# Four H banks in turn for the first four chunks of block 1, and up-projection (1,4) issued ahead of down-projection (1,0)

## The chip, the cores and the metric

One core of one Trainium2 chip runs the whole program. The metric is the device time of one execution in microseconds (us), of which less is better. The kernel is written for the separate engines of the core: PE (TensorE, matrix products into PSUM), DVE (VectorE), ACT (ScalarE), POOL (GpSimd, which reads and writes SBUF only here) and SP (SyncE, which issues the DMAs). Each engine works through its own list of instructions in order, and they meet at semaphores.

## The reference

Attention over channels is followed by two feed-forward networks (FFNs) over 6016 tokens of 256 channels, with a hidden width of 2048 in both.

```python
s = kn.transpose(0, 2, 1) @ qn / tau          # 256 x 256, softmax of its rows -> a
x = v @ a                                     # 6016 x 256
h = x @ w_in1                                 # first FFN
P = a0 + a1*h + a2*h**2 + a3*h**3
Q = 1 + abs(b0)*abs(h) + abs(b1)*h**2
x = (P / (Q + 1e-6)) @ w_out1
h = x @ w_in2                                 # second FFN
out = (h * clip(h + 3, 0, 6) / 6) @ w_out2
```

## The kernel before

**Tiling.** The tokens are cut into 12 blocks: 11 of 512 tokens and a last one of 384. The hidden width of 2048 is cut into 16 chunks of 128. A pair such as (1,4) is block 1, chunk 4. The softmax result is folded into the first FFN's up weights, so that the first FFN starts from v itself. Each product is made of three matmuls (high by high, high by low, low by high half of the operands, lines 476 to 478), for each of two halves of 128 channels, so one up- or down-projection of a chunk is a group of six matmuls.

**The four groups.** `up1(t, j)` makes a chunk of the first FFN's hidden layer in a bank of the PSUM tensor H. ACT makes the terms of Q and the start of P from it (`q_terms`, lines 804 and 806; `p_start`, line 812). DVE goes on with P in place in the same bank (`horner_2`, line 999; `horner_1`, line 1006), then makes the high half of the quotient (`quotient_hi`, line 1014), a product (`product`, line 1034) and the remainder (`rest`, line 1042). `rest` is the last to read the H bank, and its semaphore `rest_done` sets the bank free. ACT takes the reciprocal root and squares it between (`root`, line 819, and `root_squared`, line 825), after POOL has added up Q (`q_body`, line 423). POOL makes the low half (`quotient_lo`, line 429), for which `down1` (into the PSUM tensor YP) waits. When all 16 chunks of a block are down, `yT_split` (ACT line 846, then DVE line 1060) copies YP to SBUF as two halves, and only then may `down1` of the next block write YP. For the second FFN `up2(b, j)` writes H, `c1` (ACT, line 831), `gate2` (DVE, line 1048) and `c2` (ACT, line 838) read it, POOL splits the result (line 437), and `down2` adds it up in OP.

**Order.** All engines walk through slots (t, j), 16 slots for each block. In slot (t, j) PE issues `up2` of chunk j - 4 of block t - 1, `down2` two chunks behind that, `up1(t, j)`, and `down1` of the chunk three before j. The order is fixed in the program. In slots (1,0) to (1,3) there is no second FFN yet; `up2(0,0)` comes in slot (1,4), and `down2(0,0)` in slot (1,6). The one exception before is slot (1,2), where `down1(0,15)` goes ahead of `up1(1,2)`. On ACT a slot (1, j) with j of 4 and more runs `c1`, `root` and `root_squared` of chunk j - 1, `q_terms`, `p_start`, `c2`. On DVE it runs `gate2`, `quotient_hi`, `product` and `rest` of chunk j - 1, then `horner_2` and `horner_1` of chunk j. Slot (1,3) has `yT_split(0)` at its start on both.

**The H banks.** H has four banks, 0 to 3. In block 0 `up1` takes all four in turn. From block 1 on `up1` takes banks 0 and 1, and `up2` banks 2 and 3. Who waits for which bank stands in `wait_h1` and `wait_h2`; these two, `h1` and `step` of PE are what the change touches. Before, `up1(1,2)` waits for `rest(1,0)`, `up1(1,3)` for `rest(1,1)`, and `up2(0,0)` and `up2(0,1)` for `rest(0,14)` and `rest(0,15)`.

Of the kernel before, what the change touches and what calls it, by code (L numbers as in the profile page):

```python
# [28 lines left out]
def attention_ffn_ffn(nc, q, k, v, tau, w_in1, w_out1, a, b, w_in2, w_out2, out):  # L29
# [3 lines left out]
    J = F // P  # L33
# [18 lines left out]
    LAG_DOWN1 = 3  # L52
# [44 lines left out]
    with ctx:  # L97
# [75 lines left out]
        def first_folded(i, c):  # L173
# [27 lines left out]
        g1_hi_done, product_done, rest_done, g1_lo_done, d1_done = map(  # L201
            sem, ("g1_hi_done", "product_done", "rest_done", "g1_lo_done", "d1_done"))
# [11 lines left out]
        def width(blk):  # L214
            return P * (tiles_of[blk] if isinstance(blk, int) else BT)
# [5 lines left out]
        def exists(blk):  # L221
            return not isinstance(blk, int) or 0 <= blk < NB

        def chunk(t, at):

            return t + at // J, at % J

        def count(blk, j):

            return blk * J + (j + 1)  # L230

        def back(blk, j, n):

            blk, j = blk + (j - n) // J, (j - n) % J
            return None if isinstance(blk, int) and blk < 0 else (blk, j)

        def wait_chunk(engine, semaphore, at):
            if at is not None:
                engine.wait_ge(semaphore, count(*at))
# [20 lines left out]


        def h1(t, j):
            turn = 4 if isinstance(t, int) and t == 0 else 2
            return H[:, j % turn, 0:width(t)]

        def wait_h1(engine, t, j):
            if isinstance(t, int) and t == 0:
                if j >= 4:
                    wait_chunk(engine, rest_done, (0, j - 4))
            elif isinstance(t, int) and t == 1 and j < 2:  # L270
                wait_chunk(engine, rest_done, (0, J - 4 + j))
            else:
                wait_chunk(engine, rest_done, back(t, j, 2))

# [2 lines left out]

        def wait_h2(engine, blk, j):
            if isinstance(blk, int) and blk == 0 and j < 2:
                wait_chunk(engine, rest_done, (0, J - 2 + j))  # L280
            else:
                wait_chunk(engine, g2_done, back(blk, j, 2))

# [12 lines left out]
        def slot(t, j):  # L296
            return t * J + j if isinstance(t, int) else None

        def stage(t, at):

            blk, j = chunk(t, at)
            return (blk, j) if exists(blk) else None
# [170 lines left out]
        def _(pe):  # L473
            def split_product(psum, w_hi, w_lo, x_hi, x_lo, first, last):

                nc.tensor.matmul(psum, w_hi, x_hi, start=first, stop=False)  # L476
                nc.tensor.matmul(psum, w_hi, x_lo, start=False, stop=False)  # L477
                return nc.tensor.matmul(psum, w_lo, x_hi, start=False, stop=last)  # L478
# [71 lines left out]
            def fold_first(i, c):  # L550
                for d in range(CT):
                    done = nc.tensor.matmul(first_folded(i, c), probT[:, d, c * P:(c + 1) * P],
                                            w_raw_a[:, d, i * P:(i + 1) * P], start=(d == 0), stop=(d == CT - 1))
                done.then_inc(first_made, 1)
# [26 lines left out]
            def up1(t, j, par):  # L581
                w = width(t)
                wait_h1(pe, t, j)
                if j == 0:
                    pe.wait_ge(vT_lo_done, CT * (t + 1))
                cols = slice(j * P, (j + 1) * P)
                for c in range(CT):
                    if isinstance(t, int) and t == 0 and j < 2:
                        pe.wait_ge(first_lo, CT * j + c + 1)
                    elif isinstance(t, int) and t == 0 and j in PIECE_AT:  # L590
                        pe.wait_ge(fold_lo, PIECE_AT.index(j))
                    done = split_product(h1(t, j), wf_hi[:, c, cols], wf_lo[:, c, cols],
                                         vT_hi[par][:, c, 0:w], vT_lo[par][:, c, 0:w], c == 0, c == CT - 1)
                done.then_inc(u1_done, 1)

            def down1(blk, j):
                w = width(blk)
                wait_chunk(pe, g1_lo_done, (blk, j))
                if j % 4 == 0 and isinstance(blk, int) and blk == 0:
                    pe.wait_ge(wd1_lo_done, j // 4 + 1)  # L600
                for d in range(CT):
                    if j == 0 and exists(blk - 1):
                        pe.wait_ge(yT_lo_done, CT * (blk - 1) + d + 1)
                    done = split_product(YP[:, d, 0:w], wd1_hi[:, j, d * P:(d + 1) * P],
                                         wd1_lo[:, j, d * P:(d + 1) * P], g1_hi[:, j % 4, 0:w],
                                         g1_lo[:, j % 4, 0:w], j == 0, j == J - 1)
                done.then_inc(d1_done, 1)

            def up2(blk, j):
                w = width(blk)  # L610
                wait_h2(pe, blk, j)
                if isinstance(blk, int) and blk == 0 and j in (0, J // 2):
                    pe.wait_ge(wu2_lo_done, 4 if j == 0 else 8)
                cols = slice(j * P, (j + 1) * P)
                for c in range(CT):
                    if j == 0:
                        pe.wait_ge(yT_lo_done, CT * blk + c + 1)
                    done = split_product(h2(blk, j), wu2_hi[:, c, cols], wu2_lo[:, c, cols],
                                         yT_hi[:, c, 0:w], yT_lo[:, c, 0:w], c == 0, c == CT - 1)
                done.then_inc(u2_done, 1)  # L620
# [70 lines left out]
            def step(t, par):  # L691
                for j in range(J):
                    if x := stage(t - 1, j - SHIFT2):
                        up2(*x)
                    if x := stage(t - 1, j - SHIFT2 - LAG_DOWN2):
                        if isinstance(x[0], int) and x[0] == NB - 1:
                            down2_by_tokens(*x)
                        else:
                            down2(*x)
                    last_of_0 = slot(t, j) == J + LAG_DOWN1 - 1  # L700
                    if last_of_0:

                        down1(0, J - 1)
                    if exists(t):
                        up1(t, j, par)
                        if slot(t, j) == 0:

                            pe.wait_ge(probT_scaled, 1)
                            fold_first(1, 1)
                        if isinstance(t, int) and t == 0 and j in PIECE_AT[:-1]:  # L710
                            fold(PIECE_AT.index(j) + 1)
                    if not last_of_0 and (x := stage(t, j - LAG_DOWN1)):
                        down1(*x)

            every_step(pe, step)
# [422 lines left out]
```

## Time and profile before

| | |
|---|---|
| median of three runs | 1111.23 us (1110.48 to 1111.71) |
| profiled execution, device time | 1110.4 us |
| its span, first to last instruction | 1108.6 us |
| PE busy | 1093.8 us, 99% of the span |
| DVE, ACT, POOL busy | 895.8, 866.3 and 776.1 us |
| chain of work that ended last | PE 92%, DVE 4%, all else under 2% each |

The profile is one execution. Its page has the busy time of each engine, the span in 40 slices with the granted clock of PE, and the chain that ended last; the trace behind it has every instruction with its start, its length, and what ended the idle time before it. Times in the trace are counted from the start of the span. Matmuls overlap: each is shown with some 0.39 us, but the next one starts about 0.23 us after it. So the start of the next group is where a group ends for PE, and the end of its last matmul is where others may read the result. DVE, ACT and POOL instructions overlap a little too, when nothing is waited for between them.

### The profile page before, as it was taken

The page shows a single profiled execution, that of the slowest core. Times are in us where ns is not written, and L with a number is a line of the kernel's source. Part 1 is how long each engine was busy: PE and PEld are TensorE (multiplying, and loading weights), DVE is VectorE, ACT ScalarE, POOL GpSimd, SP SyncE. Part 2 cuts the span into 40 slices and gives each one's busy share as a digit, 9 for nine tenths or more (in the row PEclk, how much of TensorE's full clock was granted, in tenths as well). Part 3 has the DMA queues.
Part 4 walks back from the last instruction along what each step waited for, and adds up shares of the span by engine and source line. Part 5 has one row for each costly group of instructions (what it writes and reads, how often), then busy time and mean ns, then how long its engine had stood idle before and what let it go on. Part 6 is the DMA issues. An engine that isn't in the chain of part 4 may idle for free.

```text
span 1108.6 us, 15700 instructions
## 1 busy us (share of the span) xinstructions
PE 1093.8 (99%) x4966; PEld 914.2 (82%) x4966; DVE 895.8 (81%) x1288; ACT 866.3 (78%) x1461; POOL 776.1 (70%) x624
## 2 busy tenths in 40 slices
PE   9999799999999999999999999999999999999998
PEld 8877588888888888888888888888888888888888
DVE  6799988888888788798788788788888888877742
ACT  6799878877877877787787788788787787777744
POOL 0489878777677777777777667777777767776653
PEclk9999999999999999999999999999999999999999
DMA  9941000011011011011011011002001001001010
GB/s 348 321 119 20 0 16 5 1 20 20 1 20 20 1 20 20 1 19 19 0 19 19 1 20 20 1 2 35 3 1 20 15 1 20 0 2 20 1 20 15
DMA packets 105472, 33.92 MB, mean 31 GB/s; under 512 B 92982, under 2 KB 98742, under 8 KB 105398
## 3 DMA queue, kind: packets, MB, share of 16 engines
q1 hardware_dynamic: 104960, 32.65, 11.8%
q8 instruction: 33, 0.54, 0.2%
q14 instruction: 41, 0.34, 0.1%
q10 hardware_dynamic: 438, 0.39, 0.1%
HBM read 26.87 MB, written 6.16 MB: 30 GB/s over the span
## 4 chain that ended last, share of the span: by engine, by line
PE 92%; DVE 4%; POOL 1%; issue 1%; ACT 0%; DMA 0%; SPq 0%; DVEq 0%; ACTq 0%
PE H L476 15%; PE H L477 15%; PE H L478 15%; PE OP L477 7%; PE OP L478 7%; PE OP L476 7%; PE YP L476 7%; PE YP L477 7%; PE YP L478 7%; PE OP L507 3%; DVE H L1006 1%; DVE T L999 1%; DVE g_hi L1014 1%; DVE SQ L1042 1%; PE OP L676 1%
## 5 line engine op out<-in xcount | busy, mean ns | idle before, releaser
L423 POOL TENSOR_TENSOR SQ<-SQ,AB 128x512 f32<-128x512 f32 (+1 forms) x175 | 224.2, 1281 | 251.2 <-ACT SQ L806 251.2
L437 POOL TENSOR_TENSOR g_lo<-R,g_hi 128x512 fp32r<-128x512 f32 (+1 forms) x191 | 243.6, 1275 | 23.7 <-ACT g_hi L838 22.6
L429 POOL TENSOR_TENSOR g_lo<-SQ,Y 128x512 fp32r<-128x512 f32 (+1 forms) x192 | 245.0, 1276 | 8.6 <-DVE SQ L1042 7.9
L804 ACT ACTIVATE AB<-H,absb 128x512 f32<-128x512 f32 (+1 forms) x175 | 118.9, 680 | 145.3 <-PE H L478 145.2
L999 DVE TENSOR_TENSOR T<-T,H 128x512 f32<-128x512 f32 (+1 forms) x192 | 129.0, 672 | 80.0 <-ACT T L812 79.5
L1014 DVE SCALAR_TENSOR_TENSOR g_hi<-H,coef,Y 128x512 fp32r<-128x512 f32 (+1 forms) x192 | 141.5, 737 | 57.6 <-ACT Y L825 57.2
L476 PE MATMUL YP<-g_hi,wd_hi 128*128 128x512 f32 (+1 forms) x384 | 149.3, 389 | 4.7 <-POOL g_lo L429 4.3
L476 PE MATMUL H<-vT_hi,wf_hi 128*128 128x512 f32 (+1 forms) x384 | 149.2, 388 | 4.8 <-DVE wf_lo L969 2.5
L831 ACT ACTIVATE R<-H 128x512 f32<-128x512 f32 (+1 forms) x192 | 113.5, 591 | 50.4 <-PE H L478 50.4
L1048 DVE SCALAR_TENSOR_TENSOR R<-R,H 128x512 f32<-128x512 f32 (+1 forms) x192 | 128.1, 667 | 29.8 <-ACT R L831 28.3
L1006 DVE SCALAR_TENSOR_TENSOR H<-T,coef,H 128x512 f32<-128x512 f32 (+1 forms) x192 | 143.0, 745 | 6.8
L478 PE MATMUL H<-vT_hi,wf_lo 128*128 128x512 f32 (+1 forms) x384 | 148.0, 385 | 0.0
L478 PE MATMUL H<-yT_hi,wu_lo 128*128 128x512 f32 (+1 forms) x384 | 147.9, 385 | 0.0
L812 ACT ACTIVATE T<-H,coef 128x512 f32<-128x512 f32 (+1 forms) x192 | 147.9, 770 | 0.0
L477 PE MATMUL H<-yT_lo,wu_hi 128*128 128x512 f32 (+1 forms) x384 | 147.9, 385 | 0.0
L477 PE MATMUL H<-vT_lo,wf_hi 128*128 128x512 f32 (+1 forms) x384 | 147.8, 385 | 0.0
L478 PE MATMUL YP<-g_hi,wd_lo 128*128 128x512 f32 (+1 forms) x384 | 147.8, 385 | 0.0
L477 PE MATMUL YP<-g_lo,wd_hi 128*128 128x512 f32 (+1 forms) x384 | 147.8, 385 | 0.0
L476 PE MATMUL H<-yT_hi,wu_hi 128*128 128x512 f32 (+1 forms) x384 | 147.8, 385 | 0.0
L1042 DVE SCALAR_TENSOR_TENSOR SQ<-H,coef,SQ 128x512 f32<-128x512 f32 (+1 forms) x192 | 142.0, 740 | 6.7 <-POOL SQ L417 0.5
L1034 DVE SCALAR_TENSOR_TENSOR SQ<-SQ,g_hi 128x512 f32<-128x512 f32 (+1 forms) x176 | 139.1, 791 | 6.1
L477 PE MATMUL OP<-g_lo,wd_hi 128*128 128x512 f32 x352 | 137.0, 389 | 0.0
(123 smaller groups left out, 2070.8 us busy)
## 6 DMA issues: line engine op xcount, KB each, us to landing
qk<-in_q SPq DMA_DIRECT2D x22, 256.0 KB, 5.6
qk<-in_k SPq DMA_DIRECT2D x22, 256.0 KB, 6.3
out<-o_tok SPq DMA_DIRECT2D x88, 64.0 KB, 1.9
v_blocks<-in_v SPq DMA_DIRECT2D x80, 64.0 KB, 2.3
wd_raw<-in_moe_w_out SPq DMA_DIRECT2D x8, 512.0 KB, 8.2
wu_raw<-in_moe_w_in SPq DMA_DIRECT2D x4, 512.0 KB, 8.0
w_raw_a<-in_moe_w_in SPq DMA_DIRECT2D x2, 1024.0 KB, 10.7
v_blocks<-in_v SPq DMA_DIRECT2D x1, 512.0 KB, 6.8
```

The source lines that it names most:

```text
L423: nc.gpsimd.tensor_tensor(SQ[:, j % 4, 0:w], SQ[:, j % 4, 0:w], AB[:, j % 2, 0:w], ALU.add)\
L429: nc.gpsimd.tensor_tensor(g1_lo[:, j % 4, 0:w], SQ[:, j % 4, 0:w], Y[:, j % 2, 0:w], ALU.mult)\
L437: nc.gpsimd.tensor_tensor(g2_lo[:, j % 4, 0:w], R[:, j % 2, 0:w], g2_hi[:, j % 4, 0:w].bitcast(fp32), ALU.subtract).then_inc(g2_lo_done, 1)
L476: nc.tensor.matmul(psum, w_hi, x_hi, start=first, stop=False)
L477: nc.tensor.matmul(psum, w_hi, x_lo, start=False, stop=False)
L478: return nc.tensor.matmul(psum, w_lo, x_hi, start=False, stop=last)
L812: nc.scalar.activation(T[:, j % 2, 0:w], h1(t, j), ACT.Identity, bias=A2, scale=A3)\
L999: nc.vector.tensor_tensor(T[:, j % 2, 0:w], T[:, j % 2, 0:w], h1(t, j), ALU.mult)\
L1006: nc.vector.scalar_tensor_tensor(h, T[:, j % 2, 0:w], A1, h, ALU.add, ALU.mult).then_inc(t3_done, 1)
L1014: nc.vector.scalar_tensor_tensor(g1_hi[:, j % 4, 0:w], h1(blk, j), A0, Y[:, j % 2, 0:w], ALU.add, ALU.mult).then_inc(g1_hi_done, 1)
L1034: nc.vector.scalar_tensor_tensor(SQ[:, j % 4, 0:w], SQ[:, j % 4, 0:w], Q_CONST, g1_hi[:, j % 4, 0:w].bitcast(fp32), ALU.add, ALU.mult).the ...
L1042: nc.vector.scalar_tensor_tensor(SQ[:, j % 4, 0:w], h1(blk, j), A0, SQ[:, j % 4, 0:w], ALU.add, ALU.subtract).then_inc(rest_done, 1)
```

## The change

The first FFN keeps four H banks in turn for chunks 0 to 3 of block 1 too. So `up1(1,2)` and `up1(1,3)` write banks 2 and 3, and wait for `rest(0,14)` and `rest(0,15)`. `up1(1,4)` and `up1(1,5)` write banks 0 and 1 again, and wait for `rest(1,0)` and `rest(1,1)`. `up2(0,0)` and `up2(0,1)`, whose banks are 2 and 3, now wait for `rest(1,2)` and `rest(1,3)`. On PE `up1(1,4)` moves from slot (1,4) to slot (1,3), between `up1(1,3)` and `down1(1,0)`, and the exception of slot (1,2) is gone: `up1(1,2)` goes ahead of `down1(0,15)`. The other engines' lists are what they were, but for the bank that they address; no instruction is added or taken away.

```diff
         def h1(t, j):
-            turn = 4 if isinstance(t, int) and t == 0 else 2
+            turn = 4 if isinstance(t, int) and (t == 0 or (t == 1 and j < 4)) else 2
             return H[:, j % turn, 0:width(t)]
 
         def wait_h1(engine, t, j):
             if isinstance(t, int) and t == 0:
                 if j >= 4:
                     wait_chunk(engine, rest_done, (0, j - 4))
-            elif isinstance(t, int) and t == 1 and j < 2:
+            elif isinstance(t, int) and t == 1 and j < 4:
                 wait_chunk(engine, rest_done, (0, J - 4 + j))
+            elif isinstance(t, int) and t == 1 and j < 6:
+                wait_chunk(engine, rest_done, (1, j - 4))
             else:
                 wait_chunk(engine, rest_done, back(t, j, 2))
...
         def wait_h2(engine, blk, j):
             if isinstance(blk, int) and blk == 0 and j < 2:
-                wait_chunk(engine, rest_done, (0, J - 2 + j))
+                wait_chunk(engine, rest_done, (1, 2 + j))
             else:
                 wait_chunk(engine, g2_done, back(blk, j, 2))
...
-                    last_of_0 = slot(t, j) == J + LAG_DOWN1 - 1
-                    if last_of_0:
-
-                        down1(0, J - 1)
-                    if exists(t):
+                    if exists(t) and slot(t, j) != J + 4:
                         up1(t, j, par)
...
-                    if not last_of_0 and (x := stage(t, j - LAG_DOWN1)):
+                    if slot(t, j) == J + 3:
+
+                        up1(t, 4, par)
+                    if x := stage(t, j - LAG_DOWN1):
                         down1(*x)
```

## Rows read from the trace of the kernel before

**Rows 1.** The page, granted TensorE clock in 40 slices of the span, in tenths.

```profile
PEclk9999999999999999999999999999999999999999
```

**Rows 2.** Waits of PE over the whole span: total us, times, longest us.

```profile
PE YP L476 <- POOL g_lo L429: 4.3, 5, 1.7
...
PE H L476 <- DVE SQ L1042: 2.3, 1, 2.3
```

**Rows 3.** Stretch from 134.2 us on: length, then busy us of PE, PEld, DVE, ACT, POOL.

```profile
134.20:1108.00 973.80, 970.92 (x4410) 814.16 (x4410) 781.75 (x1117) 752.22 (x1286) 696.41 (x559) 1.00 0.07 12
```

**Rows 4.** PE's timeline, slots (1,1) to (1,5): start us, length us, line, operation, [idle before].

```profile
117.52 0.40 PE L478 MATMUL YP<-g_hi,wd_lo 128*128 128x512 f32 x1
119.65 0.50 PE L476 MATMUL YP<-g_hi,wd_hi 128*128 128x512 f32 x1 [1.73 <-POOL g_lo L429]
...
121.17 0.39 PE L476 MATMUL H<-vT_hi,wf_hi 128*128 128x512 f32 x1
...
124.97 0.50 PE L476 MATMUL H<-vT_hi,wf_hi 128*128 128x512 f32 x1 [2.29 <-DVE SQ L1042]
...
127.04 0.47 PE L476 MATMUL YP<-g_hi,wd_hi 128*128 128x512 f32 x1 [0.41 <-DVE yT_lo L1060]
...
128.50 0.40 PE L476 MATMUL H<-yT_hi,wu_hi 128*128 128x512 f32 x1
...
129.65 0.39 PE L478 MATMUL H<-yT_hi,wu_lo 128*128 128x512 f32 x1
129.88 0.40 PE L476 MATMUL H<-vT_hi,wf_hi 128*128 128x512 f32 x1
...
134.22 0.50 PE L476 MATMUL H<-vT_hi,wf_hi 128*128 128x512 f32 x1
...
135.73 0.39 PE L476 MATMUL YP<-g_hi,wd_hi 128*128 128x512 f32 x1
```

**Rows 5.** DVE's timeline of the same stretch.

```profile
117.50 0.75 DVE L1042 SCALAR_TENSOR_TENSOR SQ<-H,coef,SQ 128x512 f32<-128x512 f32 x1 [0.24 <-POOL SQ L417]
...
118.94 1.20 DVE L1034 SCALAR_TENSOR_TENSOR SQ<-SQ,g_hi 128x512 f32<-128x512 f32 x1
120.18 0.75 DVE L1042 SCALAR_TENSOR_TENSOR SQ<-H,coef,SQ 128x512 f32<-128x512 f32 x1
...
126.21 1.28 DVE L1060 TENSOR_TENSOR yT_lo<-YP,yT_hi 128x512 fp32r<-128x512 f32 x2
...
128.18 0.69 DVE L1034 SCALAR_TENSOR_TENSOR SQ<-SQ,g_hi 128x512 f32<-128x512 f32 x1
128.91 0.75 DVE L1042 SCALAR_TENSOR_TENSOR SQ<-H,coef,SQ 128x512 f32<-128x512 f32 x1
...
130.95 0.68 DVE L1048 SCALAR_TENSOR_TENSOR R<-R,H 128x512 f32<-128x512 f32 x1
131.90 0.75 DVE L1014 SCALAR_TENSOR_TENSOR g_hi<-H,coef,Y 128x512 fp32r<-128x512 f32 x1 [0.26 <-ACT Y L825]
...
133.41 0.75 DVE L1042 SCALAR_TENSOR_TENSOR SQ<-H,coef,SQ 128x512 f32<-128x512 f32 x1
```

**Rows 6.** ACT's timeline of the same stretch.

```profile
121.32 0.63 ACT L819 ACTIVATE Y<-SQ 128x512 f32<-128x512 f32 x1 [1.90 <-POOL SQ L423]
121.99 0.63 ACT L825 ACTIVATE Y<-Y 128x512 f32<-128x512 f32 x1
122.72 0.69 ACT L804 ACTIVATE AB<-H,absb 128x512 f32<-128x512 f32 x1
...
130.08 0.60 ACT L831 ACTIVATE R<-H 128x512 f32<-128x512 f32 x1 [0.92 <-PE H L478]
```

**Rows 7.** POOL's timeline of the same stretch.

```profile
118.33 1.27 POOL L429 TENSOR_TENSOR g_lo<-SQ,Y 128x512 fp32r<-128x512 f32 x1 [0.86 <-DVE SQ L1042]
...
121.26 1.29 POOL L429 TENSOR_TENSOR g_lo<-SQ,Y 128x512 fp32r<-128x512 f32 x1
...
128.56 1.47 POOL L423 TENSOR_TENSOR SQ<-SQ,AB 128x512 f32<-128x512 f32 x1 [0.72 <-ACT SQ L806]
```

## Prediction

> **What bounds the kernel now.** I read the page first. PE is the bound, and its granted clock is at the higher level (2.4 GHz) in all 40 slices [rows 1], so what counts is the time in which PE stands still. Then I asked for PE's waits over the whole span. The two largest causes are the low half of the first FFN's quotient from POOL (4.3 us in 5 waits, longest 1.7) and `rest` on DVE (2.3 us in one wait) [rows 2]. Next I asked where they lie. From 134.2 us to the end PE is busy 970.9 of 973.8 us [rows 3], and what is missing is the tail after its last matmul: no wait of PE stands there. This matters in both directions. What the change takes off or puts on before 134.2 us reaches the end in full, for nothing later gives it back.
>
> So all is decided in slots (1,1) to (1,5). In PE's timeline [rows 4] the last matmul of `down1(0,14)` starts at 117.52. PE is then ready at 117.75, and `down1(0,15)` starts at 119.65. `up1(1,2)` starts at 121.17, `up1(1,3)` at 124.97 after an idle time of 2.29, `down1(1,0)` at 127.04 after 0.41, `up2(0,0)` at 128.50, `up1(1,4)` at 129.88, `up1(1,5)` at 134.22, `down1(1,2)` at 135.73. A group of six matmuls in a run takes 129.88 - 128.50 = 1.38. One that starts from a standstill takes 135.73 - 134.22 = 1.51.
>
> The other engines are the reason for the standstills. On DVE the two halves of `yT_split` (126.21) and the ops around them follow one another with no idle mark, and `gate2(0,0)` (130.95), `quotient_hi(1,3)` (131.90, 0.26 idle), `rest(1,3)` (133.41) fill its slot [rows 5]. In this stretch DVE paces PE, and only after it PE is the bound.
>
> **The first part: `up1` in four banks.** `up1(1,2)` now waits for `rest(0,14)`, which lies before `rest(0,15)` at 117.50 in DVE's list [rows 5]. So it starts at 117.75, in the hole before `down1(0,15)`, and ends at 119.1. `down1(0,15)` keeps its start of 119.65, since its release is the POOL op at 118.33 + 1.27 = 119.60 [rows 7], which depends on nothing that moved. It lasts to 121.17. `up1(1,3)` waits for `rest(0,15)`, over at 118.25, so it starts at 121.17 instead of 124.97. `up1(1,4)` waits for `rest(1,0)`, over at 120.18 + 0.75 = 120.93 [rows 5], and starts at 122.55. PE has then done at 123.9 what it had done before at 126.5, plus one more group: it is ahead by 2.6 + 1.4 = 4.0 us. On paper this is the gain.
>
> **Why the others don't follow.** ACT's next piece of work is `root(1,1)` at 121.32, for which it waited 1.90 us on POOL's `q_body(1,1)` [rows 6]. In POOL's list that op stands between the low halves at 118.33 and 121.26 [rows 7], and no H bank releases it. So ACT stays where it is until `root_squared(1,1)` at 121.99. Only then does `q_terms(1,2)` profit. Two ops in a row on ACT, without a wait, stand some 0.54 apart, so it starts at 122.53 instead of 122.72 [rows 6]. That is 0.19 us for ACT. DVE gets nothing of it: it works without a mark of idleness up to `yT_split` at 126.21 [rows 5], and its releases come in time. So `yT_lo` is ready when it was, `down1(1,0)` starts at 127.04 as before [rows 4], and the lead is spent in one wait from 123.9 to 127.04, some 3.1 us. At 127.04 all that is left of it is that `up1(1,4)` is done already, a group of 1.38.
>
> **The second part: `up2` behind `rest`.** The waits that this adds are for `rest(1,2)` and `rest(1,3)`. Behind them on PE queue all later groups, and ACT's `c1`, DVE's `gate2` and all that follows in their lists wait for `up2`.
> - `down1(1,0)` ends at 128.50. `rest(1,2)` is at 128.91 to 129.66 [rows 5], for `quotient_hi(1,2)` and `product(1,2)` still stand behind `yT_split`. `up2(0,0)` starts at 129.71 instead of 128.50, 1.21 later. It starts from a standstill, which adds 0.12, so its last matmul ends at 129.65 + 0.39 + 1.33 = 131.37.
> - `c1(0,0)` on ACT waits for just that: before, it was idle for 0.92 and started at 130.08, directly after 129.65 + 0.39 [rows 4, 6]. It is now at 131.40. `root(1,3)` and its square are behind it in ACT's list, and `quotient_hi(1,3)` already waited 0.26 for them [rows 5], so all of the 1.33 passes to `quotient_hi(1,3)` and `rest(1,3)`. `rest(1,3)` moves from 133.41 to 134.74 and ends at 135.49.
> - `down1(1,1)` has its inputs and ends near 132.6. `up2(0,1)` comes next and waits for `rest(1,3)`: it starts at 135.54, after another idle time of 2.9. Before, the group behind `rest(1,3)` was `up1(1,5)` (134.16 to 134.22), and `up2(0,1)` had been done already. Now both lie behind it: 135.54 + 1.51 + 1.38 = 138.43 is the start of `down1(1,2)`, instead of 135.73 [rows 4].
>
> The difference is 2.70 us: 1.33 for the later `rest(1,3)` and 1.38 for the group that used to lie ahead of it. At that point PE has done the same work in both kernels. Of the 1.38 that `up1(1,4)` had gained nothing is left either: it is in the wait of 2.9 before `up2(0,1)`.
>
> **After it.** From slot (1,6) on the banks are those of before, PE has four groups in a slot, and `rest(1,4)`, `rest(1,5)`, `g2_lo(0,0)` come in time, since PE's slot there is longer than DVE's. No DMA and no queue of SP is moved, and the loads of v have no part in this stretch. No instruction is added, so nothing else has a price. The sum is made against the profiled execution: 1110.4 + 2.7 = 1113.1. That execution lies 0.8 below the median of the runs shown, 1111.23, so on the median I say 1113.9.
>
> **Bounds.** The order of POOL and DVE is the part that the trace shows only by likeness. `product` stretched to 1.20 at 118.94, where a POOL op was running (118.33 to 119.60), and it ended 0.54 after that op [rows 5, 7]. It took 0.69 at 128.18, with POOL's `q_body(1,3)` starting 0.38 later, at 128.56. After the change ACT is 0.19 earlier, so `q_body(1,3)` starts at 128.37, still 0.19 behind the product. I take the price as nothing, by the row at 128.18. The other end is 1.1 us: a POOL op of 1.27 started just ahead of the product at 128.17 would end at 129.44, the product at 129.98 instead of 128.87. Below, a gain of some tenths is possible if `yT_split` or the squares come a little earlier.
>
> **The rivals.**
> - *The rotation pays.* The waits for a bank go, ACT and DVE follow the earlier `up1`, and the idle times of 2.29, 0.41 and 1.38 out of the hole of 1.9 before `down1(0,15)` are filled: about -4.1, so 1107.1. It speaks for it that `up1(1,2)` and `up1(1,3)` are 3.4 and 3.8 us earlier. Against it are the 1.90 us that ACT waited for POOL at 121.32 and the DVE ops without idle time [rows 5, 6]. It decides if `rest(1,2)` comes before 128.5. Chance 0.05. The Trainium skill has a rule for this side ("Perfetto Trace Analysis", Optimizing Tensor Performance): independent groups of matmuls should go round different PSUM banks, so that one is emptied while the next is computed. The rule counts banks only; here each bank given to `up1` is one for which `up2` waits.
> - *Half of it.* `rest(1,3)` doesn't move, because `c1(0,0)` or the 0.26 us of slack take up the delay, and only the group behind it costs: +1.4, so 1112.6. Chance 0.13.
> - *The product falls behind POOL*, the upper bound above: +1.1 on the forecast, 1115.0. Chance 0.10.
> - *The clock falls.* PE stands still for 3.1, 1.2 and 2.9 us within 12 us; the longest standstill before was 2.3 us at the higher level [rows 1, 4]. If it went to the lower level of 1.2 GHz, each group would take 1.4 more. For `down1(1,0)` and `down1(1,1)` waits cover that; `up2(0,0)`, `up2(0,1)` and `up1(1,5)` would pay: +1.4 to +4.1 on the forecast, 1115.3 to 1118.0. Chance 0.06. The Trainium skill ("TensorE: Matmul & The Clock Gate", HAM oscillation) says that long idle gaps between bursts bring the clock down to this level; no row here shows it doing so.
> - The forecast itself has 0.66.
>
> **How the numbers follow.** A measurement of this kernel tells about 0.2% from no change, 2.2 us, so slower begins at 1113.45. The forecast's own range is 1113.2 to 1114.8, and a fifth of it falls under that bound. Slower is then 0.53 + 0.10 + 0.06 = 0.69, same is 0.13 + 0.12 = 0.25, and faster is 0.05 and a little for what I don't see, 0.06. The range reaches down to 1112.0 to hold the half case, and up to 1115.8 to hold the product behind POOL and the mild end of the clock: outside are 0.05 of the first rival and 0.05 of the last, and some scatter.
>
> **What the profile after would show.** `up1(1,2)` at 117.75 and `up1(1,3)` at 121.2; a wait of PE for `yT_lo` of about 3.1 us that ends at 127.04; two new waits for `rest` (DVE, line 1042) of about 1.2 and 2.9 us; `gate2(0,0)` at 132.0 instead of 130.95; the start of `down1(1,2)` at 138.4; no other wait after it. I am wrong if `rest(1,2)` is well before 129.7, if `quotient_hi(1,3)` doesn't move by 1.3, or if PE shows waits past 140 us.

## The result, and the profile after

| | before | after |
|---|---|---|
| median of 11 runs each, us | 1111.28 | 1114.88 |
| lowest and highest, us | 1110.43, 1112.74 | 1114.16, 1115.96 |
| ratio, 95% interval | | 1.0033 (1.0025 to 1.0040) |
| profiled execution, us | 1110.4 | 1114.37 |
| its span, us | 1108.6 | 1112.6 |

The change makes the kernel 3.6 us slower by the medians, and the profiled execution 4.0 us. Nothing in the matmuls themselves is new: PE's work, 4966 matmuls, is the same. First the page of the kernel after, its row of the granted clock in 40 slices:

```profile
PEclk9999899999999999999999999999999999999999
```

One slice, the fifth (111 to 139 us), is no longer at the full level of [rows 1]. Then the waits of PE over the whole span (total us, times, longest us; `L1061` is DVE's `yT_split`, `L431` POOL's `quotient_lo`, `L1043` `rest`):

```profile
PE YP L478 <- DVE yT_lo L1061: 3.0, 1, 3.0
PE YP L478 <- POOL g_lo L431: 2.9, 5, 0.7
PE H L478 <- DVE SQ L1043: 2.5, 2, 1.6
```

Against [rows 2], POOL's low half costs 1.4 us less (4.3 to 2.9): the hole before `down1(0,15)` has gone from 1.73 to 0.38. `rest` costs about the same (2.3 to 2.5), but in two waits and before other groups. The one wait for `yT_lo`, of 0.41 us before [rows 4], has grown to 3.0 us. PE's timeline shows where each lies (every row is the first matmul of a group, but the one at 134.62, which is the last matmul of `down1(1,1)`):

```profile
117.77 0.40 PE L478 MATMUL H<-vT_hi,wf_hi 128*128 128x512 f32 x1
...
119.69 0.50 PE L478 MATMUL YP<-g_hi,wd_hi 128*128 128x512 f32 x1 [0.38 <-POOL g_lo L431]
...
121.18 0.40 PE L478 MATMUL H<-vT_hi,wf_hi 128*128 128x512 f32 x1
...
122.56 0.39 PE L478 MATMUL H<-vT_hi,wf_hi 128*128 128x512 f32 x1
...
127.09 0.47 PE L478 MATMUL YP<-g_hi,wd_hi 128*128 128x512 f32 x1 [3.00 <-DVE yT_lo L1061]
...
129.76 0.79 PE L478 MATMUL H<-yT_hi,wu_hi 128*128 128x512 f32 x1 [0.95 <-DVE SQ L1043]
...
132.49 0.63 PE L478 MATMUL YP<-g_hi,wd_hi 128*128 128x512 f32 x1
...
134.62 0.63 PE L480 MATMUL YP<-g_hi,wd_lo 128*128 128x512 f32 x1
136.85 0.50 PE L478 MATMUL H<-yT_hi,wu_hi 128*128 128x512 f32 x1 [1.60 <-DVE SQ L1043]
...
139.72 0.39 PE L478 MATMUL YP<-g_hi,wd_hi 128*128 128x512 f32 x1
```

These are `up1(1,2)`, `down1(0,15)`, `up1(1,3)`, `up1(1,4)`, `down1(1,0)`, `up2(0,0)`, `down1(1,1)` (first and last matmul), `up2(0,1)`, `down1(1,2)`. Up to 129.76 each is within 0.05 us of the prediction. `up2(0,0)` is the first that isn't as worked out: it takes 132.49 - 129.76 = 2.73 instead of 1.51, and each matmul is shown with 0.63 us and more instead of 0.39. The stretches of 2 us say why. Their columns are stretch, length, then busy us of PE, PEld, DVE, ACT, POOL with the number of instructions, the granted clock, the DMA share and GB/s:

```profile
128.00:130.00 2.00, 1.05 (x5) 0.47 (x4) 1.93 (x4) 0.99 (x2) 1.60 (x1) 0.61 0.00 0
130.00:132.00 2.00, 2.00 (x5) 1.58 (x6) 1.06 (x2) 0.00 (x0) 1.29 (x2) 0.50 0.00 0
132.00:134.00 2.00, 2.00 (x6) 1.55 (x5) 0.65 (x1) 1.24 (x3) 0.00 (x0) 0.50 0.00 0
134.00:136.00 2.00, 1.25 (x3) 0.43 (x2) 1.48 (x3) 2.00 (x4) 0.27 (x1) 0.69 0.00 0
136.00:138.00 2.00, 1.15 (x5) 0.97 (x6) 1.93 (x4) 0.84 (x2) 2.00 (x2) 1.00 0.00 0
```

The granted clock fell to 0.50, the level of 1.2 GHz, soon after 128 us, after PE had stood still for 3.0 us and done one group, and it was back at 1.00 by 136. On ACT and DVE the late end of `up2(0,0)` goes on as `c1(0,0)`, `gate2(0,0)`, `quotient_hi(1,3)` and `rest(1,3)`:

```profile
132.72 0.60 ACT L832 ACTIVATE R<-H 128x512 f32<-128x512 f32 x1 [3.74 <-PE H L480]
```

```profile
133.35 0.69 DVE L1049 SCALAR_TENSOR_TENSOR R<-R,H 128x512 f32<-128x512 f32 x1 [2.26 <-ACT R L832]
134.53 0.75 DVE L1015 SCALAR_TENSOR_TENSOR g_hi<-H,coef,Y 128x512 fp32r<-128x512 f32 x1 [0.49 <-ACT Y L826]
...
136.05 0.75 DVE L1043 SCALAR_TENSOR_TENSOR SQ<-H,coef,SQ 128x512 f32<-128x512 f32 x1
```

In [rows 6] ACT waited 0.92 us for `up2(0,0)`; here it waits 3.74, and DVE, which had 0.26 of idle time in the same place [rows 5], has 2.26 and 0.49. `rest(1,3)` is at 136.05, 2.64 later than before: 1.33 as predicted, and 1.31 that are put down to the clock here and tested below. PE then has no wait to the end, so the 3.99 us by which `down1(1,2)` is late (139.72 against 135.73 in [rows 4]) are the 4.0 us of the span.

**A yardstick.** Whole traces begin this stretch up to 1.0 us earlier or later. Part of that is the load stage: PE's wait for the DMA of `in_k` at the start is 0.6 us in the trace of before, and 1.6 and 1.4 in the two traces that lie latest. So in what follows a trace is measured from the start of `down1(0,15)`, the last group that nothing here moves, to a later group. To `down1(1,2)` it is 135.73 - 119.65 = 16.08 before and 139.72 - 119.69 = 20.03 after. To `up1(1,6)` it was 139.83 - 119.65 = 20.18 before, and to `up1(1,7)` 145.27 - 119.65 = 25.62. To the end of the span it is 1108.6 - 119.65 = 989.0 before and 1112.6 - 119.69 = 992.9 after; this one holds all that comes later, too.

### The profile page after: what moved, and what is told of

Its sections match the earlier page's. It is cut to its first block, busy times and chain, and to the rows that moved or that the text cites. A ratio compares the mean times of both kernels' runs of the same rounds, so it can differ in the third digit from the quotient of the medians.

```text
span 1112.6 us, 15700 instructions
## 1 busy us (share of the span) xinstructions
PE 1096.6 (99%) x4966; PEld 916.7 (82%) x4966; DVE 896.1 (81%) x1288; ACT 866.0 (78%) x1461; POOL 776.2 (70%) x624
## 4 chain that ended last, share of the span: by engine, by line
PE 92%; DVE 5%; POOL 1%; issue 1%; ACT 1%; DMA 0%; SPq 0%; DVEq 0%; ACTq 0%
PE H L478 15%; PE H L480 15%; PE H L479 15%; PE OP L480 7%; PE OP L479 7%; PE OP L478 7%; PE YP L480 7%; PE YP L479 7%; PE YP L478 7%; PE OP L509 3%; DVE H L1007 1%; DVE g_hi L1015 1%; DVE T L1000 1%; DVE SQ L1043 1%; PE OP L678 0%
## 5 line engine op out<-in xcount | busy, mean ns | idle before, releaser
L431 POOL TENSOR_TENSOR g_lo<-SQ,Y 128x512 fp32r<-128x512 f32 (+1 forms) x192 | 244.7, 1274 | 8.6 <-DVE SQ L1043 7.9
L1043 DVE SCALAR_TENSOR_TENSOR SQ<-H,coef,SQ 128x512 f32<-128x512 f32 (+1 forms) x192 | 142.0, 740 | 6.7 <-POOL SQ L419 0.5
L480 PE MATMUL OP<-g_hi,wd_lo 128*128 128x512 f32 x352 | 137.2, 390 | 0.0
```

What stands on the lines that cost most here:

```text
L431: nc.gpsimd.tensor_tensor(g1_lo[:, j % 4, 0:w], SQ[:, j % 4, 0:w], Y[:, j % 2, 0:w], ALU.mult)\
L1043: nc.vector.scalar_tensor_tensor(SQ[:, j % 4, 0:w], h1(blk, j), A0, SQ[:, j % 4, 0:w], ALU.add, ALU.subtract).then_inc(rest_done, 1)
```

## The experiments

The theory now had two parts: 2.7 us of waits (1.33 and 1.38), and 1.3 us of lowered clock behind the first standstill. The idle-time matmuls used below write a bank of OP that nobody reads before it is begun anew; nothing of the kernel's computation is left out in any of these kernels. Line numbers in the rows differ from kernel to kernel, since lines were added above them. Each median comes from 5 to 11 runs. They fell on three chips, each with runs of the kernel before. Its median over those runs with a mean granted clock of 0.999 or 1.0 is the fairer one to set beside a kernel whose clock stays up:

| chip | kernels | before: runs, median | of them at 0.999 or 1.0: runs, median | the others: runs, median |
|---|---|---|---|---|
| A | first standstill filled, move undone, both `up2` in OP without and with fill | 24, 1111.47 | 9, 1110.45 | 15, 1111.95 |
| B | before filled, all filled, one `up2` in OP (two kernels) | 33, 1111.55 | 12, 1110.89 | 21, 1111.66 |
| C | nine-three-nine, first left open, more made ahead (two kernels) | 27, 1111.30 | 14, 1110.82 | 13, 1111.70 |

**One standstill filled.**

```diff
             fold_first(1, 0)
 
+            def hold_clock(n):
+
+                for _ in range(n):
+                    nc.tensor.matmul(OP[:, 0, :], wf_hi[:, 0, 0:P], vT_hi[1][:, 0, :], start=True, stop=True)
+
...
                         up1(t, 4, par)
+                        hold_clock(12)
                     if x := stage(t, j - LAG_DOWN1):
                         down1(*x)
```

> The changed kernel with twelve more matmuls of 128x512 on PE, between up1(1,4) and down1(1,0), whose result nobody reads: they take 12 x 0.23 = 2.7 us of the standstill of 3.0 us that the changed kernel has there. Theory (two terms of waits, 2.7 us, and 1.3 us of lowered clock behind that standstill): the granted clock stays at the higher level throughout, up2(0,0) takes 1.5 us instead of 2.7, rest(1,3) starts at 134.7 instead of 136.05, down1(1,2) at 138.4 instead of 139.7, and the kernel is 2.7 us slower than before instead of 4.0 (median 1113.9, ratio 1.0024). Rival (the 1.3 us has another cause, and the clock only goes with it): 1114.9 or more, since work was added.

Measured: ratio to before 1.0038 (1.0025 to 1.0052), median of 5 runs 1115.9. The median was not as the theory wanted: it lies on the rival's side of 1114.9. The profiled execution was as the theory had it, to the tenth; PE's timeline in it (idle matmuls, `down1(1,0)`, `up2(0,0)`, `up2(0,1)`, `down1(1,2)`):

```profile
123.87 2.88 PE L696 MATMUL OP<-vT_hi,wf_hi 128*128 128x512 f32 x12
127.06 0.47 PE L478 MATMUL YP<-g_hi,wd_hi 128*128 128x512 f32 x1 [0.30 <-DVE yT_lo L1067]
...
129.73 0.50 PE L478 MATMUL H<-yT_hi,wu_hi 128*128 128x512 f32 x1 [1.07 <-DVE SQ L1049]
...
135.55 0.50 PE L478 MATMUL H<-yT_hi,wu_hi 128*128 128x512 f32 x1 [2.81 <-DVE SQ L1049]
...
138.41 0.39 PE L478 MATMUL YP<-g_hi,wd_hi 128*128 128x512 f32 x1
```

Here the clock stayed up, `down1(1,2)` is 18.75 after `down1(0,15)`, 2.67 more than before, and the span is 1111.2. `up2(0,0)` takes 1.49, and DVE's row of `rest(1,3)` is back where the prediction had it (134.74), though matmuls were added and the program's waits are those of the change:

```profile
134.75 0.75 DVE L1049 SCALAR_TENSOR_TENSOR SQ<-H,coef,SQ 128x512 f32<-128x512 f32 x1
```

So the 1.31 of the change is the clock. The five runs fall in two groups: 1113.1 twice with a mean granted clock of 0.999, and 1115.9 to 1117.1 three times with 0.997 and 0.998. So the waits are worth what was worked out, and filling one standstill doesn't keep the clock: another one of 2.81 us is left ahead of `up2(0,1)`. That the clock fell behind that one in the long runs fits the later kernels, in which it is filled; those runs themselves have no trace, so it is not shown.

**The move undone.**

```diff
-                    if exists(t) and slot(t, j) != J + 4:
+                    if exists(t):
                         up1(t, j, par)
...
-                    if slot(t, j) == J + 3:
-
-                        up1(t, 4, par)
```

> The changed kernel with up1(1,4) back in its old place behind up2(0,0); the four banks and the waits of up2 for rest(1,2) and rest(1,3) stay. Theory (the lead of up1(1,4) is lost in the wait for rest(1,3)): down1(1,2) still comes behind rest(1,3), up2(0,1) and up1(1,5), so the time is that of the changed kernel, 1114.9, at most 0.6 more where the lowered clock lasts longer. Rival (the move is worth a group of 1.4 us, and without it the banks alone cost more): 1116.3.

Measured: 1.0029 (1.0018 to 1.0040), median 1114.55, the same as the change within the intervals. The lead of a group had brought nothing that the time shows. The trace has `down1(1,0)` and `up2(0,1)` at:

```profile
127.97 0.77 PE L478 MATMUL YP<-g_hi,wd_hi 128*128 128x512 f32 x1 [4.38 <-DVE yT_lo L1058]
...
137.30 0.50 PE L478 MATMUL H<-yT_hi,wu_hi 128*128 128x512 f32 x1 [1.43 <-DVE SQ L1040]
```

The standstill ahead of `down1(1,0)` grows by the group to 4.38, and the one ahead of `up2(0,1)` still ends with `rest(1,3)`. The clock is at 0.50 here too, but earlier, from 126 to 132, and back at 1.00 from 134 on, so that `down1(1,2)` comes 140.16 - 120.57 = 19.59 after the mark, 0.44 less than in the change. With the clock up this kernel wasn't run; that the move is worth nothing there rests on `up2(0,1)` ending behind `rest(1,3)` either way.

**Both `up2` without their waits.** The two banks of OP are free until `down2(0,0)`; DVE has read the last of bank 1 with the sum of chunk (1,0), whose semaphore is `w_done`, and `down2(0,0)` now waits until `gate2` has read the two banks.

```diff
+        def in_op(blk, j):
+            return isinstance(blk, int) and blk == 0 and j in (0, 1)
+
         def h2(blk, j):
+            if in_op(blk, j):
+                return OP[:, j, 0:width(blk)]
             return H[:, 2 + j % 2, 0:width(blk)]
 
         def wait_h2(engine, blk, j):
-            if isinstance(blk, int) and blk == 0 and j < 2:
+            if in_op(blk, j):
+                wait_chunk(engine, w_done, (1, 0))
+            elif isinstance(blk, int) and blk == 0 and j < 2:
                 wait_chunk(engine, rest_done, (1, 2 + j))
...
                 for d in range(CT):
+                    if j == 0 and in_op(blk, d):
+                        wait_chunk(pe, g2_done, (0, d))
```

> The changed kernel with up2(0,0) and up2(0,1) in the two banks of OP, which are free there, so that neither waits for rest(1,2) or rest(1,3); all else as changed. Theory: both waits for rest go, up2(0,0) starts near 128.5, but still behind the standstill of 3 us and so at the lower clock. Its end is 1.3 us later than before, rest(1,4) too, and up1(1,6), which waits for that, starts within 0.3 us of its old 139.8: the time is that of the kernel before, within 0.4 us (1110.9 to 1111.6). Rival (the waits for rest are not what costs): above 1113.5.

Measured: 0.9995 (0.9986 to 1.0004), median 1110.95. In its trace the clock is at 0.51 from 130 to 132, and `up1(1,6)` is 20.37 after `down1(0,15)`, 0.19 more than before. The waits for `rest` are what costs, and in this trace the lowered clock alone eats the group made ahead. The 11 runs are of two kinds, though the program is one and nothing is filled: five with a mean clock of 1.0 lie at 1109.80 to 1110.04 (median 1109.87), six with 0.998 at 1110.95 to 1112.60 (median 1111.5). The median of 1110.95 is the lowest run of the second kind, so that it fell into the expected range is luck. The long runs are like the trace, where the clock fell behind the standstill of 3.0 us; in the others it stayed up, as far as the mean tells. So such a standstill can bring the clock down, and doesn't do it every time. With the first standstill filled as well:

> As up2_in_op, and the twelve matmuls of fill in the standstill before down1(1,0). Theory: no wait of up2 and no lowered clock; up1(1,4) made ahead of time is then worth its group: up1(1,6) starts at 138.4, when rest(1,4) is done, 1.4 us earlier than before, and the kernel takes 1109.9 (ratio 0.9987). Rival (what was made ahead is lost in a later wait anyway): 1111.2.

Measured: 0.9986 (0.9977 to 0.9995), median 1109.85 of 11 runs, all between 1109.2 and 1110.9 at a mean clock of 0.999 or 1.0.

```profile
119.67 0.50 PE L485 MATMUL YP<-g_hi,wd_hi 128*128 128x512 f32 x1 [0.39 <-POOL g_lo L438]
...
138.46 0.50 PE L485 MATMUL H<-vT_hi,wf_hi 128*128 128x512 f32 x1 [0.23 <-DVE SQ L1058]
```

`up1(1,6)` comes after 18.79, 1.39 less than before. The next group that waits gives a part back: `up1(1,7)` is at 144.18 - 119.67 = 24.51, 1.11 less than before, and to the end of the span it is 987.9, 1.0 less. That is the gain of the group made ahead; the ratio of 0.9986 holds some of the kernel before's lowered clock, too, and against its runs at 0.999 or 1.0 (1110.45) the median gains 0.6. The median is also that of the five runs without fill whose clock stayed up (1109.87), so here the twelve matmuls themselves cost nothing. A group made ahead pays once `up2` isn't behind `rest` and the clock is kept.

**The kernel before with its own standstills filled.** Its runs scatter, too. The nine of chip A with a mean clock of 0.999 or 1.0 have a median 1.5 us under that of the other fifteen; on chips B and C the same difference is 0.8 and 0.9.

```diff
             def step(t, par):
                 for j in range(J):
+                    if slot(t, j) == J + 2:
+                        hold_clock(7)
+                    if slot(t, j) == J + 3:
+                        hold_clock(9)
                     if x := stage(t - 1, j - SHIFT2):
                         up2(*x)
```

> The kernel before, with seven idle-time matmuls of 128x512 ahead of down1(0,15) and nine ahead of up1(1,3), where PE stands still for 1.9 and 2.4 us; nobody reads their result. Theory (part of the kernel's scatter is the clock, which in some runs falls behind these standstills too; the lowest runs, 1110.3, are those in which it doesn't): nothing on the path moves, and all runs lie at 1110.3 to 1110.9, median 1110.5, about 0.9 under the kernel before. Rival (the scatter has another source): median 1111.4 and the same scatter.

Measured: 0.9993 (0.9984 to 1.0002), median 1110.51, all of 11 runs between 1110.4 and 1111.3. The median moved as the theory has it and the scatter narrowed, but the interval of the ratio holds 1, so for the time itself this is not settled. The mean clock is 0.999 or 1.0 in every run. In the trace `down1(1,2)` is 135.55 - 119.48 = 16.07 after the mark, as before.

**All standstills of the change filled,** with twelve ahead of `down1(1,0)`, four ahead of `up2(0,0)`, eleven ahead of `up2(0,1)`.

> The changed kernel with PE kept busy in all three standstills: twelve such matmuls ahead of down1(1,0), four ahead of up2(0,0), eleven ahead of up2(0,1). In the kernel with the first twelve alone the profiled execution was as expected (span 1111.2, down1(1,2) at 138.41), but most timed runs were 2.8 to 4.0 us longer at a lower mean clock. Theory (the waits cost 2.7 us; what comes on top is the clock, which can also fall behind the second and third standstill): all runs at 1113.0 to 1113.7, and 2.7 us over the kernel before with its own standstills filled. Rival (the waits alone cost what was measured, 3.6): 1114.5 or more.

Measured: 1.0022 (1.0013 to 1.0031), median 1113.99, 1112.9 to 1114.5, mean clock 0.999 or 1.0 in all 11 runs. The median is 0.3 us above the expected range, between theory and rival, and it is 3.5 us over the kernel before filled, not 2.7 (3.1 over the kernel before's twelve runs at 0.999 or 1.0). By the medians alone the theory isn't borne out. In the trace the stretch is as worked out, 138.40 - 119.64 = 18.76, and more stands far behind it: a pause of 0.5 us before a matmul of `up1` at 458.65, for which the trace names no engine. The span has it, too (1112.0).

```profile
PE H L478 <- issue: 0.5, 1, 0.5
```

**The same with nine, three and nine.**

> fill_all with fewer idle-time matmuls: nine, three and nine instead of twelve, four and eleven. fill_all lay at 1114.0, 0.9 over the 1113.1 that the two terms give, though its down1(1,2) came at 138.40 as worked out. Theory (the waits cost 2.7 and the rest is not in this stretch; a pause of 0.5 us without a waited-for engine stood in its trace near 440 us): 1113.2 to 1114.0. Rival (the added matmuls themselves cost what is over): under 1113.5, in proportion to their number, 0.7 instead of 0.9.

Measured: 1.0021 (1.0012 to 1.0030), median 1113.42, 1113.2 to 1114.1, with 139.19 - 120.44 = 18.75 in its trace and no such pause. Both statements had room for this number, so it doesn't tell them apart. It is 2.6 over the kernel before's runs at 0.999 or 1.0 on the same chip (1110.82). The stretch itself is the same to 0.01 us whatever the number of idle matmuls, so they are not on the path there.

**Only the first standstill left open.**

> The changed kernel with its second and third standstills filled (four and eleven matmuls), the first one, 3.0 us ahead of down1(1,0), left open. Theory (the clock falls behind the first standstill): the granted clock is at the lower level from near 128.5 on, up2(0,0) takes 2.7 us, rest(1,3) comes near 136, and down1(1,2) at 139.7, where the changed kernel has it: median 1114.9, 0.9 over fill_all. Rival (it is the sum of the three that brings the clock down): 1114.0, as fill_all.

Measured: 1.0037 (1.0024 to 1.0051), median 1114.8 of 5 runs, all with a mean clock of 0.998 or less; that is 1.4 over the kernel with all three filled on the same chip (1113.42). The clock in stretches of its trace (columns as above):

```profile
128.00:130.00 2.00, 2.00 (x8) 1.63 (x7) 1.93 (x4) 1.52 (x3) 1.38 (x2) 0.71 0.00 0
130.00:132.00 2.00, 2.00 (x6) 1.52 (x6) 1.58 (x3) 0.00 (x0) 1.83 (x2) 0.50 0.00 0
132.00:134.00 2.00, 2.00 (x10) 1.60 (x9) 0.22 (x1) 0.85 (x2) 0.00 (x0) 0.94 0.00 0
```

It falls in the same place as in the change, behind the one standstill of 3.0 us, though PE was kept busy directly after it. `down1(1,2)` comes after 140.14 - 120.22 = 19.92, 1.17 more than with all three filled, so the number is as expected, but the way to it is not: the four idle matmuls at the lowered clock end late and put off `up2(0,0)`, which starts 10.76 after the mark instead of 10.07, and it then takes 132.95 - 130.98 = 1.97, not 2.7. So the first standstill can be enough: in this kernel all 5 runs have the lower mean clock, in the one with both `up2` in OP 6 of 11. Whether the gaps behind it make a fall more frequent was not tested.

**One wait at a time.** Here `up2(0,0)` alone is in OP, so only `up2(0,1)` waits; the standstills are filled.

> The changed kernel with up2(0,0) alone in a free bank of OP, so that only up2(0,1) still waits, for rest(1,3); the standstills ahead of down1(1,0) and of up2(0,1) are filled with twelve matmuls each. Theory (two terms: 1.33 because up2(0,0) waits and so delays rest(1,3), 1.38 because up2(0,1) stands behind rest(1,3)): rest(1,3) back at 133.4, up2(0,1) at 134.2, down1(1,2) at 137.1, so 1.4 us over the kernel before with its standstills filled, 1111.9. Rival (both terms come from the wait of up2(0,0)): 1110.5.

Measured: 1.0010 (1.0001 to 1.0019), median 1112.29. `down1(0,15)` and `down1(1,2)` in its trace:

```profile
120.08 0.50 PE L485 MATMUL YP<-g_hi,wd_hi 128*128 128x512 f32 x1 [0.37 <-POOL g_lo L438]
...
137.52 0.39 PE L485 MATMUL YP<-g_hi,wd_hi 128*128 128x512 f32 x1
```

That is 17.44, 1.36 more than before: the second term alone. The median is 1.8 above the kernel before filled, and 1.4 above the kernel before's runs at 0.999 or 1.0. Then the other way round, `up2(0,1)` alone in OP:

> The changed kernel with up2(0,1) alone in a free bank of OP, so that only up2(0,0) still waits, for rest(1,2); the standstills ahead of down1(1,0) and up2(0,0) are filled with twelve and four matmuls. Theory: rest(1,3) is still at 134.7, but no group of PE waits for it, down1(1,2) comes at 135.3, and the next to wait is up1(1,6), for rest(1,4) at 139.7, where it started before too (139.83). So the delay of 1.33 costs nothing by itself: 1110.4 to 1110.6. Rival (the terms simply add, and this one costs its 1.3): 1111.8.

Measured: 0.9996 (0.9987 to 1.0005), median 1111.19, in the middle between theory and rival: 0.7 above the kernel before filled, 0.3 above the kernel before's runs at 0.999 or 1.0. The trace tells them apart. It has `down1(0,15)` at 120.64, late from the load stage, and then

```profile
130.72 0.50 PE L485 MATMUL H<-yT_hi,wu_hi 128*128 128x512 f32 x1 [0.17 <-DVE SQ L1060]
...
140.76 0.50 PE L485 MATMUL H<-vT_hi,wf_hi 128*128 128x512 f32 x1 [0.23 <-DVE SQ L1060]
```

`up2(0,0)` waits as in the change, yet `up1(1,6)` is at 20.12 after the mark, 0.06 less than before. To the end of the span it is 0.3 more than before: `up1(1,7)`, at 146.48 - 120.64 = 25.84, is 0.22 later, behind a `product(1,5)` of 1.67 us (of which more below). So the delay of `rest(1,3)` by 1.33 costs at most 0.3 unless a group of PE stands behind it, and the two terms are not two causes that add: the first counts only because of the second.

**A version that makes more ahead.** From the kernel with both `up2` in OP:

```diff
-                    if exists(t) and slot(t, j) != J + 4:
+                    if slot(t, j) == J + 6:
+
+                        down1(1, 3)
+                    if exists(t) and slot(t, j) not in (J + 4, J + 5):
                         up1(t, j, par)
...
                         up1(t, 4, par)
-                    if x := stage(t, j - LAG_DOWN1):
+                        up1(t, 5, par)
+                    if slot(t, j) != J + 6 and (x := stage(t, j - LAG_DOWN1)):
                         down1(*x)
```

> up2_in_op (up2(0,0) and up2(0,1) in OP's two banks) with up1(1,5) made ahead too, between up1(1,4) and down1(1,0), which breaks the standstill of 3 us in two (2.4 and 1.1), and down1(1,3) ahead of up1(1,6). No idle-time matmuls. Theory (PE's list may run ahead as far as banks are free that nobody else waits for; then the next wait is rest(1,5), over at 143.1): up1(1,7) starts at 143.2 instead of 145.3, so 2.1 us less than before: lowest runs 1108.3, median 1108.3 to 1109.3 since the clock may fall behind the 2.4 us in some. Rival (DVE is the bound up to there and gives the lead back, as in the changed kernel): 1110.5 or more.

Measured: 0.9987 (0.9978 to 0.9996), median 1109.88, faster than both kernels, but by half of what was expected: 0.9 under the kernel before's runs at 0.999 or 1.0. The clock is at 0.999 or 1.0 in all runs without any idle matmul; the longest standstill between 117 and 140 is 0.94 us, where 2.4 was expected. To hold the clock without any fill is its one advantage. Over `up2` in OP with one group made ahead and the clock up (1109.87 and 1109.85) nothing is gained. Half of the expected gain is lost at `up1(1,7)`, 145.31 - 120.67 = 24.64 after the mark instead of 25.62, so 0.98 gained, where the filled kernel with one group ahead gained 1.11:

```profile
145.31 0.50 PE L485 MATMUL H<-vT_hi,wf_hi 128*128 128x512 f32 x1 [1.35 <-DVE SQ L1056]
```

It waits for `rest(1,5)`, and the op ahead of that on DVE, `product(1,5)`, began 0.05 us behind an op of POOL:

```profile
142.67 1.80 DVE L1048 SCALAR_TENSOR_TENSOR SQ<-SQ,g_hi 128x512 f32<-128x512 f32 x1
```

```profile
142.62 1.30 POOL L432 TENSOR_TENSOR SQ<-SQ,AB 128x512 f32<-128x512 f32 x1 [0.33 <-ACT SQ L820]
```

Its 1.80 us instead of 0.69 end 0.55 after POOL's op, as in [rows 5] and [rows 7] the 1.20 did, 0.54 after. The Trainium skill ("GPSIMD Engine Reference", Specifications) says that GpSimd's way into SBUF is shared with VectorE, and that instructions of VectorE with two inputs in SBUF contend with it; `product` is the only one of DVE's ops in a slot that has two, and the traces agree. In the three other kernels that have `up2(0,1)` in OP, `product(1,5)` begins 0.17 us behind the same POOL op, takes 1.67, and ends 0.55 after it, too. That PE would gain the other 1.1 us without this overlap is an estimate from 1.80 - 0.69; no kernel here has it undone. With nine idle matmuls ahead of `up1(1,5)`:

> As ahead2, with nine idle-time matmuls between up1(1,4) and up1(1,5), in the standstill of 2.4 us. Theory: the clock stays up in every run, so all runs at 1108.3 to 1109.0. Rival (a lead of PE is lost in DVE's chain): 1110.5.

Measured: 0.9989 (0.9980 to 0.9998), median 1109.91, no different from the version without them; `product(1,5)` takes 1.79 us here as well. The nine are not all idle time: they last 2.0 us where the standstill is 0.94, and `up1(1,5)` comes 126.13 - 119.88 = 6.25 after the mark instead of 5.33. That it costs nothing is since `up1(1,7)` waits for `rest(1,5)` anyway (24.72 after the mark).

**All traces by one measure,** the time from the mark to the end of the span, less the 989.0 of the kernel before. A kernel in which nothing moved, the one before filled, is at 0.2, so less than that is not told apart.

| kernel | us against before |
|---|---|
| the change | +4.0 |
| first standstill filled (clock up in the trace) | +2.6 |
| all filled; of it 0.5 the pause | +3.4 |
| nine, three and nine | +2.6 |
| only the first left open | +3.8 |
| the move undone | +3.5 |
| `up2(0,0)` alone in OP, filled | +1.4 |
| `up2(0,1)` alone in OP, filled | +0.3 |
| both in OP, clock lowered | +0.6 |
| both in OP, filled | -1.0 |
| more made ahead, without and with fill | -0.8, -0.7 |

## Why the prediction was right, and where it was not

- **The number.** 1113.9 was said, 1114.88 came. It is in the stated range of 1112.0 to 1115.8, but just outside the 1113.2 to 1114.8 that the forecast itself claimed; the range reached that far for the sake of the rivals, the clock among them. Part of the hit is luck: the 0.8 us between the trace of before and its median was added as scatter, and by the later runs that is for the most part the kernel before's own lowered clock. Without it the forecast would have been 1113.1, 1.8 under what came. On the profiled executions, 1113.1 was said and 1114.37 came, and that 1.3 is the clock.
- **The place.** That the change decides in slots (1,1) to (1,5), and nothing after gives it back, holds: after `up2(0,1)` no wait of PE stands in the trace.
- **The first part.** `up1(1,2)`, `up1(1,3)` and `up1(1,4)` went ahead as worked out, ACT followed by 0.2 us and DVE not at all, and the lead went into one wait of 3.0 us for `yT_lo` (3.1 forecast). The kernel with the move undone takes the same time, so the lead was worth nothing.
- **The second part.** 2.70 was the sum; 2.67 and 2.68 is what the traces with the clock up show. The medians of the filled kernels are less exact, 2.6 to 3.5 over the kernel before. One correction to its reading: I named two terms that add. The kernels with one wait each gave +1.36 and -0.06 in their traces (+1.4 and +0.3 to the end). The wait of `up2(0,0)` is all but free alone, and 1.33 only with `up2(0,1)` behind `rest(1,3)`.
- **The clock.** This is the step that was mis-sized: the sum put it at nothing, and it measured 1.3. It was a rival with 0.06, on the ground that 2.3 us of standstill hadn't lowered the clock in the trace of before. One of the prediction's own signs of being wrong came true by it: `quotient_hi(1,3)` moved by 2.63 (131.90 to 134.53), not by 1.3. The clock did fall, and the price was at the lower end of what was given: 1.3 us for `up2(0,0)` alone, since waits covered `down1(1,1)` and the clock was back for `up2(0,1)`. For the same reason the wait ahead of `up2(0,1)` is 1.60 and not 2.9: `down1(1,1)` ended later. All 11 runs of the change have a mean clock of 0.998 or less, so it happened in each, as far as that mean tells. The ground was weak in itself: one profiled execution is not all executions, and 49 of the 84 runs of the kernel before on the three chips have a mean clock under 0.999, too. The Trainium skill's rule ("TensorE: Matmul & The Clock Gate", HAM oscillation), that long idle gaps between bursts of matmuls bring the clock down, is the better guide here, and the trace of after agrees (0.50 behind a standstill of 3.00 us). That it doesn't happen every time is what the 11 runs with both `up2` in OP add.
- **The sum of the two.** 4.0 us in the traces and 3.6 by the medians fit together: the trace of before is an execution without the loss, 0.9 under its own median, and the trace of after is 0.5 under its own.
- **The product behind POOL** did not happen in the change (`product` 0.69 at 128.23 and 135.32), but it did, at `product(1,5)`, in each kernel with `up2(0,1)` in OP and its waits gone: 1.67 us, and 1.80 in the version that makes more ahead, 1.1 over the 0.69, the price that was given.

Two readings of the trace of before were wrong, neither with an effect on the sum. PE's second largest cause of waits is not `rest` with 2.3 us but the folded weights of the load stage, and DVE isn't without an idle mark up to `yT_split`:

```profile
PE H L476 <- DVE wf_lo L969: 2.5, 4, 1.1
```

```profile
122.65 0.75 DVE L1014 SCALAR_TENSOR_TENSOR g_hi<-H,coef,Y 128x512 fp32r<-128x512 f32 x1 [0.34 <-ACT Y L825]
```

DVE waits there for `root_squared(1,1)`, which the prediction rightly held in place by POOL's `q_body(1,1)`. So at this point it is POOL and ACT that hold DVE back, and through it PE.

## What to carry to other kernels

A buffer given to one stage is taken from another: before spreading a stage over more banks, list who waits for each bank afterwards, and what stands behind those waits on the same engine. An engine that runs ahead of a chain it later waits for gains only a longer standstill; put ahead work whose buffers nobody else needs, and read from the pacing engine's timeline whether it can follow. And count the clock of TensorE as part of the price of a long standstill, also where the profiled execution of the kernel before happened to go without. Where the runs of one kernel fall in two kinds by their mean clock, compare like with like.

## What the runs showed of the hardware that was not expected

The scatter of one kernel can be the clock. The runs of the kernel before with a mean granted clock under 0.999 were 1.5, 0.8 and 0.9 us longer by the median on the three chips, and with two standstills of about 2 us filled with idle matmuls all runs had 0.999 or 1.0 and lay within 0.9 us, where those of the unfilled kernel on the same chip lay within 2.7. The same standstill of 3.0 us lowered the mean clock in 6 of 11 runs of one program, at 1.6 us by the medians. Idle matmuls of 128x512 cost nothing where they end 0.3 us before the wait does, with the clock up; behind a standstill that had lowered it, four of them put the next group off by 0.7 us. What stays open is the pause of 0.5 us without a cause in one trace, why the clock falls in one execution and not in the next, and some 0.3 to 0.9 us by which the medians of the filled kernels lie above the sum; part of it is the load stage, which shifted whole traces by up to 1.0 us.
